# Seven block products in place of eight in the last product of an attention, expert and feed-forward kernel

## What is computed

```
x   = attention(q, k, v)              # 4 x 8 heads, 768 tokens, windowed -> [3072, 512]
x   = soft_moe(x, phi, w1, w2)        # softmax over tokens and over 32 slots, 8 experts
h   = x @ w_in                        # [3072, 512] @ [512, 2048]
g   = relu(h) ** 2
out = g @ w_out                       # [3072, 2048] @ [2048, 512]
```

## Time and profile before

| | |
|---|---|
| median of 3 runs | 565.27 us (564.38 to 565.62) |
| profiled execution | 565.99 us, of it a span of 564.0 us from the first to the last instruction |
| TensorE busy | 520.0 us, 92% of the span |
| VectorE, ScalarE, GpSimd busy | 291.5, 274.9, 107.1 us |
| mean granted clock of TensorE | 0.982 |
| feed-forward part | from 269.93 us to the end of the span |

### The profile page before, as it was taken

The page is one execution under the profiler, slowest core; times in us unless marked ns, Lnnn a source line. Parts: engine busy times, 40 slices in busy tenths (PEclk is TensorE's granted clock), DMA queues, the critical chain, the costliest instruction groups (busy, mean ns, idle before and its releaser), DMA issues.

```text
span 564.0 us, 10786 instructions
## 1 busy us (share of the span) xinstructions
PE 520.0 (92%) x3477; PEld 400.6 (71%) x3477; DVE 291.5 (52%) x909; ACT 274.9 (49%) x722; POOL 107.1 (19%) x230
## 2 busy tenths in 40 slices
PE   2899999999999688676899999999999999999997
PEld 1677877888788522311788888888888888888886
DVE  4676676676776542302797444444443543544410
ACT  1677777777877310001766443443443444444420
POOL 1444444444444203300260000000000000000000
PEclk9999999999999979797999999999999999999999
DMA  6699945535644679998001000000000000000000
GB/s 256 231 403 405 405 161 186 193 126 153 206 144 129 224 294 397 387 387 321 1 0 40 20 22 33 19 19 19 19 37 19 19 19 19 19 37 19 19 20 37
DMA packets 25993, 77.01 MB, mean 137 GB/s; under 512 B 2416, under 2 KB 2416, under 8 KB 23408
## 3 DMA queue, kind: packets, MB, share of 16 engines
q1 hardware_dynamic: 21776, 64.10, 31.6%
q10 hardware_dynamic: 4192, 12.58, 5.9%
HBM read 70.39 MB, written 6.29 MB: 136 GB/s over the span
## 4 chain that ended last, share of the span: by engine, by line
PE 69%; DVE 8%; ACT 5%; issue 5%; POOL 4%; SPq 4%; DMA 3%; ACTq 0%; DVEq 0%; POOLq 0%
PE bank L1091 14%; PE bank L1090 14%; PE bank L1089 14%; PE bank L860 5%; PE bank L871 5%; POOL probs L385 4%; ACT probs L719 4%; PE bank L1076 4%; SPq L338 4%; PE bank L903 2%; DMA w_b<-w_dram 2%; PE bank L886 2%; PE bank L1038 1%; DVE g_s L688 1%; DVE probs L478 1%
## 5 line engine op out<-in xcount | busy, mean ns | idle before, releaser
L1091 PE MATMUL bank<-wo_hi,g_lo 128*128 128x512 f32 x352 | 138.6, 394 | 0.0
L1090 PE MATMUL bank<-wo_lo,g_hi 128*128 128x512 f32 x352 | 138.1, 392 | 0.0
L1089 PE MATMUL bank<-wo_hi,g_hi 128*128 128x512 f32 x352 | 137.4, 390 | 0.0
L688 DVE TENSOR_TENSOR g_s<-relu_s 128x512 f32<-128x512 f32 x96 | 69.4, 729 | 129.5 <-ACT relu_s L814 129.5
L814 ACT ACTIVATE relu_s<-bank 128x512 f32<-128x512 f32 x96 | 56.3, 596 | 124.3 <-PE bank L1076 124.2
L719 ACT ACTIVATE probs<-probs,nmax 128x232 f32<-128x232 f32 (+1 forms) x192 | 88.6, 463 | 50.5 <-DVE nmax L478 50.5
L385 POOL TENSOR_SCALAR probs<-probs,rden 128x232 f32<-128x232 f32 (+1 forms) x192 | 82.5, 448 | 104.3 <-DVE rden L487 104.3
L1091 PEld LDWEIGHTS bank<-wo_hi,g_lo 128*128 128x128 f32 x352 | 66.2, 188 | 14.1
L1090 PEld LDWEIGHTS bank<-wo_lo,g_hi 128*128 128x128 f32 x352 | 66.1, 188 | 11.9
L1089 PEld LDWEIGHTS bank<-wo_hi,g_hi 128*128 128x128 f32 x352 | 66.2, 188 | 11.6
L691 DVE TENSOR_TENSOR g_lo<-g_s,g_hi 128x512 fp32r<-128x512 f32 x96 | 68.7, 722 | 4.5
(11 more groups left out here) (129 smaller groups left out, 507.6 us busy)
## 6 DMA issues: line engine op xcount, KB each, us to landing
qkv_s<-qkv_dram SPq DMA_DIRECT2D x16, 1028.0 KB, 5.7
qkv_s<-qkv_dram SPq DMA_DIRECT2D x16, 704.0 KB, 4.1
w_s<-w_dram ACTq DMA_DIRECT2D x5, 2048.0 KB, 11.9
w_s<-w_dram SPq DMA_DIRECT2D x6, 1024.0 KB, 13.4
out_dram<-o_stage SPq DMA_DIRECT2D x24, 256.0 KB, 2.0
w_a<-w_dram SPq DMA_DIRECT2D x9, 512.0 KB, 10.9
wo_raw<-w_out_dram SPq DMA_DIRECT2D x4, 1024.0 KB, 14.3
w_pre<-w_dram ACTq DMA_DIRECT2D x1, 2048.0 KB, 18.0
```

The lines of the kernel that those rows point to most:

```text
L688: dve.tensor_tensor(g_s[:, j % 4, :], relu_s[:, j % 4, :], relu_s[:, j % 4, :], ALU.mult).then_inc(squared, 1)
L1089: pe.matmul(bank[4 + q][:, :], hi, wo_hi[:, f, :], start=(f == 0), stop=False)
L1090: pe.matmul(bank[4 + q][:, :], hi, wo_lo[:, f, :], start=False, stop=False)
L1091: last = pe.matmul(bank[4 + q][:, :], lo, wo_hi[:, f, :], start=False, stop=(f == FFC - 1))
```

## The change

A pair of token tiles and a 2x2 split of the contraction and of the output columns are taken as 2x2 blocks: `g` has the blocks a11, a12 (first tile, lower and upper half of the features) and a21, a22 (second tile), and `w_out` four blocks of 1024 features by 256 columns. Eight block products are replaced by seven. Their operands are P0 = a11, P1 = a12, then four sums (s0 = a21+a22, s1 = s0-a11, s2 = a11-a21, s3 = a12-s1) and a22, each with a block or a sum of blocks of `w_out` (`t_32`, made once). Every matmul of these pairs has 256 columns. The sums are made in 32 bits on VectorE and split into `s_hi` and `s_lo`; a11 and a12 go to `a_hi` and `a_lo`. These have one buffer each. The seven results are put together by seven additions of 256 columns on VectorE (`outputs`), which write `o_stage`.

A pair is worked in two groups (c = 0 and 1) of a quarter of the features from each half; the group's number is G = 2k + c. In a group PE makes P0, P1, P2, four matmuls of `hidden` for group G+2, P3, P4, four more, P5 and P6. Each product is 12 matmuls. The relu and the square now both stand on ScalarE, in pieces of 1024 elements (`gate`). The first pair is done without the method (`plain`), and GpSimd no longer takes part. The other 11 pairs are done with it.

ScalarE's list, in the loop of the kernel before: two relus (bank to `relu_s`), two copies to `g_hi`, over and over, and a result copied out.

The sums and the results' additions stand in one row behind `a_lo`, where before there were only two kinds of instruction and neither read a result. The diff, cut to its core (the removed functions stand in the listing above):

```diff
+        a_hi = nc.alloc_sbuf_tensor_at("a_hi", [P, 2, GF, P], F32R, offset=REG_C + 16384)
+        a_lo = nc.alloc_sbuf_tensor_at("a_lo", [P, 2, GF, P], F32R, offset=REG_C + 16384 + 4096)
 
         logits = at(REG_D, "logits", [P, NT, SLOTS])
...
             def store(it, q):
-                sp.wait_ge(o_copied, it * 4 + (q + 1 + 4))
+                k = it * 2 + q // 2
+                sp.wait_ge(o_made, k * 7 + (6 + q % 2))
                 sp.dma_start(out_v[it * 4 + q], o_stage[:, q, :]).then_inc(out_in[q], 16)
...
-            for c in range(FFC // 2, FFC):
-                pool.wait_ge(wo_hi_done, c + 1)
-                pool.tensor_tensor(wo_lo[:, c, :], wo_raw[:, c, :], wo_hi[:, c, :].bitcast(F32), ALU.subtract)\
-                    .then_inc(wo_split_pool, 1)
...
+            def combine(c, which):
+                fs = slice(GF * c, GF * c + GF)
...
+            def wo_low(c, at):
+
+                dve.wait_ge(t_made, 4 * c + 4)
+                for m, n in enumerate((c, 2 + c)):
+                    fs = slice(4 * n, 4 * n + 4)
+                    dve.wait_ge(wo_hi_done, at + m + 1)
+                    dve.tensor_tensor(wo_lo[:, fs, :], wo_raw[:, fs, :], wo_hi[:, fs, :].bitcast(F32), ALU.subtract)\
+                        .then_inc(wo_lo_done, 1)
+
+            def t_low(c):
+                fs = slice(GF * c, GF * c + GF)
+                for j in range(4):
+                    dve.wait_ge(t_hi_done, 4 * c + j + 1)
+                    dve.tensor_tensor(t_lo[j][:, fs, :], t_32[j][:, fs, :], t_hi[j][:, fs, :].bitcast(F32), ALU.subtract)\
+                        .then_inc(t_lo_done, 1)
+
+            combine(0, (0, 1, 2))
...
+            combine(0, (3,))
...
+            wo_low(0, 0)
+
+            def blocks_low(G, c):
+
+                dve.wait_ge(hi_done, G * 6 + 1)
+                dve.tensor_tensor(a_lo[:, :, :, :], g_s[c][:, :, :, 0:P], a_hi[:, :, :, :].bitcast(F32), ALU.subtract)\
+                    .then_inc(lo_done, 1)
+
+            def slot_low(G, j, m):
+
+                dve.wait_ge(hi_done, G * 6 + m)
+                dve.tensor_tensor(s_lo[:, j, :, :], s_32[:, j, :, :], s_hi[:, j, :, :].bitcast(F32), ALU.subtract)\
+                    .then_inc(lo_done, 1)
+
+            def plain_low(c):
+                G = c
+                blocks_low(G, c)
+                dve.wait_ge(hi_done, G * 6 + 6)
+                dve.tensor_tensor(s_lo[:, 0:2, :, :], g_s[c][:, :, :, P:CH], s_hi[:, 0:2, :, :].bitcast(F32), ALU.subtract)\
+                    .then_inc(lo_done, 5)
+
+            def outputs(k, o, turn, which):
...
+                if which == 0:
+                    for t in range(2):
+                        dve.wait_ge(out_in[2 * o + t], turn * 16 + 16)
+                    dve.wait_ge(p1_copied, k)
+                    dve.tensor_tensor(o_stage[:, 2 * o, 0:HD], bank[4][:, HD:D], post[:, 0, :], ALU.add).then_inc(o_made, 1)
+                elif which == 1:
+                    dve.tensor_tensor(post[:, 1, :], bank[5][:, HD:D], post[:, 0, :], ALU.add).then_inc(o_made, 1)
+                elif which == 2:
+                    need(2)
+                    dve.tensor_tensor(post[:, 2, :], bank[6][:, 0:HD], post[:, 1, :], ALU.add).then_inc(o_made, 1)
+                    need(3)
+                    dve.tensor_tensor(o_stage[:, 2 * o + 1, HD:D], bank[5][:, 0:HD], post[:, 2, :], ALU.add).then_inc(o_made, 1)
+                    dve.tensor_tensor(post[:, 1, :], bank[5][:, 0:HD], post[:, 1, :], ALU.add).then_inc(o_made, 1)
+                    need(5)
+                    dve.tensor_tensor(o_stage[:, 2 * o, HD:D], bank[6][:, HD:D], post[:, 1, :], ALU.add).then_inc(o_made, 1)
+                else:
+                    dve.tensor_tensor(o_stage[:, 2 * o + 1, 0:HD], post[:, 2, :], bank[7][:, 0:HD], ALU.subtract).then_inc(o_made, 1)
+
+            def plain_outputs():
+                for t in range(2):
...
+            def group(k, c, o=None, turn=None):
...
+                def spent(n):
+                    dve.wait_ge(product_done, G * 7 + (n - 7))
+
+                blocks_low(G, c)
+                if c == 0 and o is not None:
+                    outputs(k - 1, o, turn, 0)
+                elif c == 0:
+                    spent(7)
+                    plain_outputs()
+                dve.wait_ge(squared, G * 2 + 2)
+                dve.sem_inc(waits_over, 1)
+                spent(3)
+                dve.tensor_tensor(s_32[:, 0, :, :], a21, a22, ALU.add).then_inc(sums_made, 1)
+                spent(4)
+                dve.sem_inc(waits_over, 1)
+                dve.wait_ge(sums_made, G * 4 - 7)
+                dve.tensor_tensor(s_32[:, 1, :, :], s_32[:, 0, :, :], a11, ALU.subtract).then_inc(sums_made, 1)
+                if c == 0 and o is not None:
+                    outputs(k - 1, o, turn, 1)
+                spent(5)
+                dve.tensor_tensor(s_32[:, 2, :, :], a11, a21, ALU.subtract).then_inc(sums_made, 1)
+                dve.wait_ge(sums_made, G * 4 - 6)
+                dve.sem_inc(waits_over, 1)
+                slot_low(G, 0, 2)
+                spent(6)
+                dve.sem_inc(waits_over, 1)
+                dve.tensor_tensor(s_32[:, 3, :, :], a12, s_32[:, 1, :, :], ALU.subtract).then_inc(sums_made, 1)
+                if c == 0 and o is not None:
+                    outputs(k - 1, o, turn, 2)
+                dve.wait_ge(sums_made, G * 4 - 4)
+                dve.sem_inc(waits_over, 1)
+                slot_low(G, 1, 3)
+                slot_low(G, 2, 4)
+                slot_low(G, 3, 5)
+                dve.wait_ge(hi_done, G * 6 + 6)
+                dve.tensor_tensor(s_lo[:, 4, :, :], a22, s_hi[:, 4, :, :].bitcast(F32), ALU.subtract).then_inc(lo_done, 1)
+                if c == 0 and o is not None:
+                    spent(7)
+                    outputs(k - 1, o, turn, 3)
+
+            plain_low(0)
+            combine(1, range(4))
+            wo_low(1, 2)
+            plain_low(1)
+            t_low(0)
+            group(1, 0)
+            t_low(1)
+            group(1, 1)
+            with dve.Fori(0, (NPAIR - 2) // 2) as it:
+                for o in range(2):
+                    k = it * 2 + (2 + o)
+                    group(k, 0, 1 - o, it + o)
+                    group(k, 1, 1 - o, it + o)
+            for which in range(4):
+                dve.wait_ge(product_done, 2 * NPAIR * 7 - 7 + (2, 4, 6, 7)[which])
...
+                act.activation(wo_hi[:, 4 * n:4 * n + 4, :], wo_raw[:, 4 * n:4 * n + 4, :], ACT.Copy).then_inc(wo_hi_done, 1)
+
+            def t_high(c):
+                fs = slice(GF * c, GF * c + GF)
+                for j in range(4):
+                    act.wait_ge(t_made, 4 * c + j + 1)
+                    act.activation(t_hi[j][:, fs, :], t_32[j][:, fs, :], ACT.Copy).then_inc(t_hi_done, 1)
...
+            def gate(G, c, first):
+
+                if not first:
+                    act.wait_ge(lo_done, G * 6 - 6)
+                    act.sem_inc(waits_act, 1)
+                for u in range(2):
+                    act.wait_ge(h_ready, G * 2 + (u + 1))
+                    act.activation(g_s[c][:, u, :, :].rearrange("p f n -> p (f n)"), banks[:, u * 1024:(u + 1) * 1024], ACT.Relu)\
+                        .then_inc(relu_done, 1)
+                for u in range(2):
+                    act.wait_ge(relu_done, G * 2 + (u + 1))
+                    act.activation(g_s[c][:, u, :, :], g_s[c][:, u, :, :], ACT.Square).then_inc(squared, 1)
+
+            def blocks_high(G, c):
+                act.wait_ge(squared, G * 2 + 2)
+                act.activation(a_hi[:, :, :, :], g_s[c][:, :, :, 0:P], ACT.Copy).then_inc(hi_done, 1)
...
+                if c == 1:
+                    act.wait_ge(product_done, 7)
+                act.activation(s_hi[:, 0:2, :, :], g_s[c][:, :, :, P:CH], ACT.Copy).then_inc(hi_done, 5)
+
+            def group(k, c, earlier=True):
+                G = k * 2 + c
+                act.wait_ge(product_done, G * 7 - 5)
+                act.sem_inc(waits_act, 1)
+                blocks_high(G, c)
+                if c == 0 and earlier:
+                    act.wait_ge(o_made, k * 7 - 7)
+                    act.activation(post[:, 0, :], bank[4][:, 0:HD], ACT.Copy).then_inc(p1_copied, 1)
+                for j in range(4):
+                    act.wait_ge(sums_made, G * 4 + (j - 7))
+                    act.activation(s_hi[:, j, :, :], s_32[:, j, :, :], ACT.Copy).then_inc(hi_done, 1)
+                act.wait_ge(product_done, G * 7)
+                act.activation(s_hi[:, 4, :, :], g_s[c][:, 1, :, P:CH], ACT.Copy).then_inc(hi_done, 1)
...
+            gate(0, 0, True)
+            plain_high(0)
+            wo_high(1)
+            wo_high(3)
+            gate(1, 1, True)
+            plain_high(1)
+            t_high(0)
+            gate(2, 0, False)
+            t_high(1)
+            gate(3, 1, False)
+            group(1, 0, False)
+            gate(4, 0, False)
+            group(1, 1, False)
```

(121 more changed lines are left out.)

149 lines of the change are left out of this document (56 added, 93 removed).

## The result

The changed kernel takes 642.82 us (642.32 to 643.82, 4 runs) against 565.44 us: a ratio of 1.137 (1.134 to 1.140). 628 us had been forecast, with a range of 604 to 655. The profiled execution has a span of 640.9 us.

What follows compares the result with a forecast made beforehand. PE issuing without a gap bounded the old kernel. Start to 332.5 us plus nine pairs at 29.3 (263.7) gave 596.2; the last pair reached 623.7, the span 627.1, the run about 628 us, range 604 to 655.

Steps and rivals of the forecast that it cites:

- The mechanism: Loop: ScalarE's `a_hi` stands behind a relu waiting for `hidden`, so PE idles about 2.5 us every group; chance 70%.
- the chain S to P0: Loop: from the start (S) of the gate's second relu to the next group's P0, 5.16 us (c = 1) or 5.50 (c = 0).
- the 4.12 that was weighed beside it: Relu to end of `a_hi` if ScalarE instructions each waited out a fixed cost: 4.12 us, not 3.85; sum 6 us higher.
- The additions: Loop, c = 0: P2 waits for VectorE's additions to free bank 5, starting 10.1 us after the second relu's start, 1.7 late.
- the 2.5 us at P0: Loop: PE stands still about 2.5 us in every group before P0, having only P5 and P6 left.
- PE's own gain: Loop pairs: 184 matmuls of 256 columns at 0.122 us, 22.4 us against 24.0; 1.6 us a pair, some 17 in all.
- The lower price: Skill page's 0.109 us per 256-column matmul: path 1.4 us a pair less, sum about 612; set aside for the trace.
- the clock in the loop: Rival: PE's stops in each loop pair lower its clock, 3.2 us a pair, 32 us in all, 660 us; chance 13%.
- The start: Before the loop: first product at 276.7 us, 3.5 late; first pair done at 300.6; group 2's P0 at 307.2 after 6.6 idle.
- The 3.0 us charged for group 2: Clock loss charged behind PE's 6.6 us wait ahead of group 2, putting its second relu at 307.2 + 8.7 + 3.0 = 318.9.
- PE stays the bound: Rival: in the loop `a_hi` is ready before P6 ends and P2's wait goes; a run at 550 us, faster; chance 5%.

Runs made afterwards that it cites:

- the warm start: Kernel with `a_hi` ahead of the gate and three additions moved forward (551.04 us), plus 26 and 18 unneeded PE matmuls in two early waits: 547.43 us.
- the first: Changed kernel with `a_hi` of the next group (with c = 0 also the copy of P0's result) ahead of the gate's relus on ScalarE: 556.80 us, ratio 0.985.
- fifth experiment: On the kernel with `a_hi` ahead of the gate, VectorE's three additions that free bank 5 stand ahead of the first `s_lo`: 551.04 us, ratio 0.977.
- the second: Changed kernel with 18 unneeded 256-column matmuls on PE behind P6 of each group up to the last pair but one: 628.92 us, ratio 1.112.
- third: Changed kernel with the copy to `a_hi` of the next group between the two relus and two squares of `gate` on ScalarE: 589.67 us, ratio 1.043.
- fourth experiment: Changed kernel with the second four `hidden` matmuls on PE behind P3 instead of P4, twelve matmuls sooner: 599.36 us, ratio 1.060.

## Why the prediction was right, and where it was off

- **The mechanism.** "ACT comes to `a_hi` only behind `gate` of group G+2" was right in place and size: the chain S to P0 was 5.17 and 5.50 us against 5.16 and 5.50. From S to the end of `a_hi` it was 3.85 us, as summed, so ScalarE's instructions did overlap and the 4.12 that was weighed beside it is refuted. Two edits at different ends of it (squares behind `a_hi`, `hidden` 12 matmuls earlier) and its removal gave 589.7, 599.4 and 556.8 us where 587, 598 and 551 were expected.
- **The additions.** P2 at S+10.1 was right, and once the clock was up its wait was 1.45 us (forecast 1.7, which like the 2.5 us at P0 is counted from start to start: 1.46 shown and 0.16).
- **PE's own gain.** 22.4 us a pair of matmuls was forecast, at 0.122; the loop without a stop takes 21.9, at 0.119 to 0.120. The method takes 2.1 us off each pair of 24.0. The lower price in the Trainium skill's page "TensorE: Matmul & The Clock Gate", section "Back-to-back issue gap" (262 cycles, an estimate of 0.109), is not reached in the loop of any run here.
- **The step that failed is the clock in the loop.** The stops of 2.4 and 2.7 us were taken as harmless after the 2.09 us stop at 271 us of the kernel before, and the case had been given 13%. In the loop they cost clock each time, twice a pair. In size that is the missing term: nine pairs at 30.72 in place of 29.3 are 12.8 of the 13.8 us by which the span was off. As a rival it had been priced at 3.2 us a pair, too high, since half of it falls where P2 waits in any case; it was 1.4. The time still fell inside the range, because that left room for it, and not because the case had been thought likely. The rule that the rival took from the Trainium skill's page "TensorE: Matmul & The Clock Gate", section "Why this matters for your kernels", that gaps between bursts of matmuls bring the slow level back, was the right side; the gaps that the page warns of are longer than these, and one of 2.38 us, at 324.7, did nothing.
- **The start.** Group 2 came 2.7 us later than forecast, because the first pair ran partly at 1.2 GHz (to 282.0) behind a 3.4 us stop that I had seen but not charged; the warm start gave 2.6 of them back. The 3.0 us charged for group 2 were in part too much (S came 9.6 behind P0, not 11.7). The clock was already back 2.9 us behind that restart, since most of the slow stretch lay inside the stop. By luck the two nearly cancel, and hide two wrong terms: pair 2's P0 was at 338.7, forecast 338.0.
- **Of the rivals,** "PE stays the bound" was wrong for this kernel but its price came close for the kernel in which the order is mended: 550 against 551.0 measured with the additions first. That too is partly luck: ten pairs at 21.9 in place of 22.4 are 5 us less, and the later start of group 2 (304.0 in place of 300.6) and the stop ahead of its P2 take them back.

## What to carry to other kernels

Put the instruction that the next product waits for ahead, in its engine's list, of those that wait for work further ahead. When one engine's list interleaves two stages, walk it from wait to wait; busy shares of 50 to 60%, as ScalarE and VectorE had here, say nothing about it. And price each stop of PE twice: its length, and what the clock costs behind it.

## What the runs showed of the hardware

- In the changed kernel's loop PE's clock went to 1.2 GHz at every one of 19 stops of 2.38 to 2.81 us between 12.5 to 13.1 us of matmuls, each time for 3.4 us, and also at a stop of 2.42 us in the first and fifth experiment. It stayed at 2.4 GHz at the changed kernel's stop of 2.38 us at 324.7, at the one of 2.09 us in the kernel before, and at all stops of up to 1.49 us in the loops of the second, third and fourth experiment. What sets a stop of 2.38 us that costs clock apart from one that does not is not shown.
- At 1.2 GHz a 256-column matmul follows the last after 0.21 us, at 2.4 GHz after 0.12.
- Matmuls that nobody needs, put into a stop, made a kernel 13.9 us faster in one case (642.82 to 628.92) and 3.6 in another (551.04 to 547.43).
- ScalarE on 1024 elements took 1.02 us from PSUM and 1.04 to 1.06 from SBUF, VectorE 1.22 to 1.23: the straight line through 512 and 768 elements held to 0.02 us, also for squares in place and for strided reads. From PSUM there is no row of 768, and the slope from SBUF was used; a line through the two PSUM rows, of 256 and 512, would have given 1.07.
